# A fused attention and two-MLP kernel: probabilities turned by a transfer in 16-bit halves instead of on the matrix engine, and one relu buffer instead of two

## The reference

```python
# attention: B, H, S, D = 2, 8, 768, 64; block, window = 32, 16
k_sum = k.reshape(B, H, nb, block, D).max(axis=3)
v_sum = v.reshape(B, H, nb, block, D).mean(axis=3)
scores_l = scale * np.matmul(q, k.transpose(0, 1, 3, 2))        # kept where |i - j| < window
scores_s = scale * np.einsum('bhsd,bhnd->bhsn', q, k_sum) + np.log(block)
a = softmax(concatenate([masked scores_l, scores_s], axis=-1))
x = np.matmul(a, concatenate([v, v_sum], axis=2))               # to (1536, 512)
# first MLP, 512 -> 2048 -> 512
h = np.maximum(x @ w_in, 0.0);  y = h * h @ w_out
# second MLP, 512 -> 1024 -> 512
h = y @ w_in2;  solu = h * softmax(h)
out = layer_norm(solu) * g_ln @ w_out2
```

## Time and profile before

| | |
|---|---|
| median of 3 runs | 466.51 us (466.35 to 466.55) |
| profiled execution | 465.99 us, span 464.2 us |
| PE busy | 455.2 us (98%) |
| DVE busy | 261.3 us (56%) |
| ACT busy | 200.9 us (43%) |
| POOL busy | 63.1 us (14%) |
| granted clock | full in all 40 slices |
| attention slots of PE | 46.7 to 236.5 us |
| second MLP | from 323.8 us |

### The profile page before, as it was taken

How to read it: one execution, slowest core, us unless ns; L and a number is a source line. 1 busy time by engine, 2 the same in 40 slices (tenths; PEclk the granted TensorE clock), 3 DMA queues, 4 the chain that set the end, 5 groups by cost and what they waited for, 6 DMA issues and landing times.

```text
span 464.2 us, 6668 instructions
## 1 busy us (share of the span) xinstructions
PE 455.2 (98%) x2526; PEld 375.1 (81%) x2526; DVE 261.3 (56%) x441; ACT 200.9 (43%) x473; POOL 63.1 (14%) x52
## 2 busy tenths in 40 slices
PE   7989999999999999999999999999999999999997
PEld 5778888888888888888888888888888888888875
DVE  4997887866644534434224234444657676767630
ACT  2988555474633433433223233333342345344411
POOL 1420000100000000000000000000135345434510
PEclk9999999999999999999999999999999999999999
DMA  8999487822103511100031111221134334453251
GB/s 284 295 288 256 160 265 227 254 66 59 56 1 111 165 35 26 40 2 1 0 92 45 45 47 49 62 70 46 47 90 58 79 68 69 91 101 82 68 114 45
DMA packets 53120, 45.99 MB, mean 99 GB/s; under 512 B 33376, under 2 KB 38112, under 8 KB 53088
## 3 DMA queue, kind: packets, MB, share of 16 engines
q1 hardware_dynamic: 53088, 45.56, 36.3%
HBM read 33.82 MB, written 5.24 MB: 84 GB/s over the span
## 4 chain that ended last, share of the span: by engine, by line
PE 94%; DVE 2%; DMA 1%; ACT 1%; issue 1%; SPq 0%; POOL 0%; ACTq 0%; DVEq 0%; POOLq 0%
PE bank L993 28%; PE bank L1021 28%; PE bank L1137 14%; PE bank L1119 14%; PE bank L913 4%; PE bank L970 3%; PE bank L938 2%; DMA q_first<-q_head 1%; ACT probs L505 1%; DVE probs L714 1%; DVE probs L696 1%; DVE neg_max L700 1%; PE bank L919 0%; ACT o_sb L661 0%; POOL k_ext L450 0%
## 5 line engine op out<-in xcount | busy, mean ns | idle before, releaser
L727 DVE TENSOR_TENSOR sqr<-relu 128x512 f32<-128x512 f32 x48 | 33.1, 690 | 99.3 <-ACT relu L563 99.3
L563 ACT ACTIVATE relu<-bank 128x512 f32<-128x512 f32 x48 | 28.7, 597 | 119.7 <-PE bank L993 119.7
L993 PE MATMUL bank<-x_hi,win_hi 128*128 128x512 f32 x192 | 76.4, 398 | 0.0
L1021 PE MATMUL bank<-h_hi,wout_hi 128*128 128x512 f32 x192 | 75.1, 391 | 0.0
L993 PE MATMUL bank<-x_hi,win_lo 128*128 128x512 f32 x192 | 74.9, 390 | 0.0
L1021 PE MATMUL bank<-h_hi,wout_lo 128*128 128x512 f32 x192 | 74.7, 389 | 0.0
L993 PE MATMUL bank<-x_lo,win_hi 128*128 128x512 f32 x192 | 74.7, 389 | 0.0
L1021 PE MATMUL bank<-h_lo,wout_hi 128*128 128x512 f32 x192 | 74.7, 389 | 0.0
L489 POOL COPY planes<-cen 128x2048 uint16<-128x2048 uint16 x12 | 33.6, 2798 | 299.8 <-PE bank L1021 244.0
L505 ACT ACTIVATE probs<-probs,neg_max 128x120 f32<-128x120 f32 x96 | 36.6, 382 | 13.5 <-DVE neg_max L700 13.4
L993 PEld LDWEIGHTS bank<-x_hi,win_lo 128*128 128x128 f32 x192 | 36.0, 188 | 7.8
(11 more groups left out here) (79 smaller groups left out, 698.3 us busy)
## 6 DMA issues: line engine op xcount, KB each, us to landing
win_raw<-w_in_t SPq DMA_DIRECT2D x8, 512.0 KB, 6.4
q_sb<-qT SPq DMA_DIRECT2D x16, 256.0 KB, 3.9
wout_raw<-w_out_t SPq DMA_DIRECT2D x8, 512.0 KB, 6.5
win_raw<-w_t SPq DMA_DIRECT2D x8, 512.0 KB, 3.6
v_ext<-vwin SPq DMA_DIRECT2D x16, 192.0 KB, 4.2
out<-o_sb SPq DMA_DIRECT2D x12, 256.0 KB, 2.8
k_ext<-kT SPq DMA_DIRECT2D x12, 192.0 KB, 3.8
k_raw<-kT SPq DMA_DIRECT2D x4, 400.0 KB, 6.0
```

The source lines that it names most:

```text
L563: nc.scalar.activation(relu[:, n % 2, :], up_bank(n), ACT.Relu).then_inc(relu_ok, 1)
L727: nc.vector.tensor_tensor(sqr[:, n % 3, :], relu[:, n % 2, :], relu[:, n % 2, :], ALU.mult)\
L993: last = nc.tensor.matmul(up_bank(n), win[a][:, f * WC + k * P:f * WC + (k + 1) * P], x[b][:, c % 2, k * CH:(k + 1) * CH], start=(k == 0 a ...
L1021: last = nc.tensor.matmul(down_bank(d), wout[a][:, f * WC + d * P:f * WC + (d + 1) * P], h[b][:, n % 3, :], start=(f == 0 and a == 0 and b ...
```

## The change

For units 10 to 23 (BY_DMA = 10, the third unit after the first chunk's eight) the four transposes on PE and the copy on ACT are taken out. In their place:

- GpSimd, `split_probs(u)`: after normalise(u) it copies the 480 float32 columns as low and high 16-bit halves into `halves`, once the transfer of unit u-1 has landed. It stands behind the windows and summaries of the same slot. `halves` has 128 columns a tile, and is cleared once at the start.
- SyncE, `turn_probs(u+2)`: at the end of iteration u, after its loads (and after spread_v at u = 10), it waits for the split and for the join of unit u+1 (for unit 10: for values(9), since `probsT_in` lies in the second half of `probsT`), and issues one transposing transfer of 128 x 1024 16-bit elements.
- DVE, `join_probs(u)`: placed after normalise(u+1) in the slot of unit u-1; it waits for the transfer and for values(u-1), and writes the first half of `probsT`, which all these units use.

Relu has one buffer instead of two: relu(n) on ACT waits for sqr(n-1) and h_hi(n-1). In the second MLP the copy o_sb of token tile 8 is put ahead of the cast lnT_hi of tile 11 instead of behind it; the other tiles keep their order.

```diff
--- before.py
+++ after.py
@@ -71,6 +71,8 @@
     return h + 2 if u % UPC == 0 and u >= 2 * UPC else h
 
 
+
+BY_DMA = UPC + 2
 X_AT = {x_half(u): u for u in range(UPC, UNITS)}
 
 K_AT = {1: 0, 3: 1, 5: 2, 6: 3}
@@ -132,7 +134,7 @@
         parts.close()
         wout_hi = sb(ctx, "wout_hi", [P, F1 * WC], F32R)
         hid = ExitStack()
-        relu = sb(hid, "relu", [P, 2, CH], F32)
+        relu = sb(hid, "relu", [P, CH], F32)
         h_hi = sb(hid, "h_hi", [P, 3, CH], F32R)
 
         squared = ExitStack()
@@ -142,7 +144,7 @@
         hid.close()
 
         o_sb = sb(ctx, "o_sb", [P, 2, DM], F32)
-        sb(ctx, "hid_rest", [P, 8 * CH - 2 * DM], F32)
+        sb(ctx, "hid_rest", [P, 7 * CH - 2 * DM], F32)
         ident = sb(ctx, "ident", [P, P + AVG], F32)
         minus_half = sb(ctx, "minus_half", [P, 1], F32)
         g_sb = sb(ctx, "g_sb", [P, F2], F32)
@@ -154,6 +156,12 @@
         v_ext = sb(att, "v_ext", [P, PPB, TPU * P], F32)
         k_sum = sb(att, "k_sum", [P, PPB, NB], F32)
         probs = sb(att, "probs", [P, 2, UC], F32)
+
+        halves = sb(att, "halves", [P, 2, TPU, P], U16)
+        turned_halves = ExitStack()
+        sb(turned_halves, "probsT_first", [P, TPU * P], F32)
+        probsT_in = sb(turned_halves, "probsT_in", [P, 2, TPU, P], U16)
+        turned_halves.close()
         probsT = sb(att, "probsT", [P, 2, TPU * P], F32)
         neg_max = sb(att, "neg_max", [P, 2, TPU], F32)
         row_sum = sb(att, "row_sum", [P, 2, TPU], F32)
@@ -198,6 +206,7 @@
         vkept_ok = sem("vkept_ok")
         scores_ok, masked_ok, max_ok, exp_ok = sem("scores_ok"), sem("masked_ok"), sem("max_ok"), sem("exp_ok")
         den_ok, rec_ok, norm_ok = sem("den_ok"), sem("rec_ok"), sem("norm_ok")
+        halves_ok, halves_in = sem("halves_ok"), sem("halves_in")
         probsT_ps, probsT_ok, attn_ps = sem("probsT_ps"), sem("probsT_ok"), sem("attn_ps")
         xhi_ok, xlo_ok = sem("xhi_ok"), sem("xlo_ok")
 
@@ -315,6 +324,17 @@
                     sp.dma_start(y_dram[0, c, :, cols], x_hi[:, c % 2, cols].bitcast(F32)).then_inc(y_saved[d], 16)
                     sp.wait_ge(yclo_ok, KD * c + d + 1)
                     sp.dma_start(y_dram[1, c, :, cols], x_lo[:, c % 2, cols].bitcast(F32)).then_inc(y_saved[d], 16)
+
+            def turn_probs(u):
+
+                sp.wait_ge(halves_ok, u - BY_DMA + 1)
+                if u == BY_DMA:
+                    sp.wait_ge(attn_ps, u)
+                else:
+                    sp.wait_ge(probsT_ok, u)
+                sp.dma_start(probsT_in[:, :, :, :].rearrange("p h t q -> p (h t) q"),
+                             halves[:, :, :, :].rearrange("p h t c -> p (h t c)"), transpose=True)\
+                  .then_inc(halves_in, 16)
 
             def load_vw_first(g):
                 h, cols = g // 2, slice((g % 2) * 2 * TPU * P, (g % 2 + 1) * 2 * TPU * P)
@@ -385,6 +405,8 @@
                     spread_v(PPB - 1)
                     load_w(wout_raw, w_out_t, F1 // WG - 1, wout_in)
                     sp.dma_start(g_sb[:, :], g_cols).then_inc(g_in, 16)
+                if u + 2 < UNITS:
+                    turn_probs(u + 2)
 
             def load_w2(g):
                 sp.wait_ge(up_ok, LAST + WG * (g + 1))
@@ -450,9 +472,17 @@
                 nc.gpsimd.tensor_copy(dst, k_sum[:, p, :].unsqueeze(1).to_broadcast([P, TPU, NB]))\
                   .then_inc(kbc_ok, 1)
 
+            def split_probs(u):
+                pool.wait_ge(norm_ok, u + 1)
+                if u > BY_DMA:
+                    pool.wait_ge(halves_in, 16 * (u - BY_DMA))
+                src = probs[:, u % 2, :].bitcast(U16).rearrange("p (t c h) -> p h t c", t=TPU, h=2)
+                nc.gpsimd.tensor_copy(halves[:, :, :, 0:KX], src).then_inc(halves_ok, 1)
+
             nc.gpsimd.memset(idle[:, 0:2 * P], 0.0).then_inc(idle_ok, 1)
             nc.gpsimd.memset(eps_sum[:, :], EPS_SUM).then_inc(eps_ok, 1)
             nc.gpsimd.memset(minus_half[:, :], -0.5).then_inc(half_ok, 1)
+            nc.gpsimd.memset(halves[:, :, :, :], 0)
             windows_k(0)
             summaries_k(0, 0)
             windows_k(1)
@@ -473,12 +503,13 @@
             windows_k(UPC + 2)
             for n in range(LAST):
                 for h in (2 * n, 2 * n + 1):
-                    if h in SLOTS and SLOTS[h][2] is not None and SLOTS[h][2] + 1 < UNITS:
+                    if h in SLOTS and SLOTS[h][2] is not None:
                         u = SLOTS[h][2] + 1
                         if UPB <= u < UPB + PPB:
                             summaries_k(1, u - UPB)
                         if u < UPB:
                             windows_k(u)
+                        split_probs(SLOTS[h][2])
 
             pool.wait_ge(half_ok, 1)
             pool.wait_ge(down_ok, STEPS)
@@ -558,13 +589,14 @@
 
             def hidden(n):
                 act.wait_ge(up_ok, n + 1)
-                if n >= 2:
-                    act.wait_ge(sq_ok, n - 1)
-                nc.scalar.activation(relu[:, n % 2, :], up_bank(n), ACT.Relu).then_inc(relu_ok, 1)
+                if n >= 1:
+                    act.wait_ge(sq_ok, n)
+                    act.wait_ge(hhi_ok, n)
+                nc.scalar.activation(relu[:, :], up_bank(n), ACT.Relu).then_inc(relu_ok, 1)
                 act.wait_ge(relu_ok, n + 1)
                 if n >= 3:
                     act.wait_ge(down_ok, n - 2)
-                nc.scalar.activation(h_hi[:, n % 3, :], relu[:, n % 2, :], ACT.Square).then_inc(hhi_ok, 1)
+                nc.scalar.activation(h_hi[:, n % 3, :], relu[:, :], ACT.Square).then_inc(hhi_ok, 1)
 
             def chunk_y(c):
                 act.wait_ge(down_ok, (c + 1) * F1)
@@ -616,7 +648,7 @@
                 for h in (2 * n, 2 * n + 1):
                     if h % 2 and n + 2 < STEPS:
                         hidden(n + 2)
-                    if h in SLOTS and SLOTS[h][1] is not None:
+                    if h in SLOTS and SLOTS[h][1] is not None and SLOTS[h][1] < BY_DMA:
                         copy_probsT(SLOTS[h][1])
                     if h in X_AT:
                         x_high(X_AT[h])
@@ -632,6 +664,14 @@
             w2_high(F1 - 2)
             w2_high(F1 - 1)
 
+            def scaled(i):
+                act.wait_ge(rstd_ok, i + 1)
+                act.wait_ge(o_ps, i + 1)
+                if i >= 2:
+                    act.wait_ge(o_out[i % 2], 16 * (i // 2))
+                nc.scalar.activation(o_sb[:, i % 2, :], bank[:, 4 + i % 2, :], ACT.Copy, scale=stat[:, i % 8, 8:9])\
+                  .then_inc(o_ok, 1)
+
             for s in range(TT + 4):
                 p, w = s % 2, s % 8
                 if s < TT:
@@ -646,6 +686,8 @@
                     act.wait_ge(cen_ok, s + 1)
                     nc.scalar.activation(solu[:, p, :], cen[:, p, :], ACT.Square, accum_out=stat[:, w, 6:7])\
                       .then_inc(var_ok, 1)
+                if s == TT:
+                    scaled(s - 4)
                 if 1 <= s <= TT:
                     if s == 1:
                         act.wait_ge(down_ok, STEPS)
@@ -653,13 +695,8 @@
                     if s >= 5:
                         act.wait_ge(o_ps, s - 4)
                     nc.scalar.copy(lnT_hi[:, (s - 1) % 4, :], lnT[:, 1 - p, :]).then_inc(lnhi_ok, 1)
-                if s >= 4:
-                    act.wait_ge(rstd_ok, s - 3)
-                    act.wait_ge(o_ps, s - 3)
-                    if s >= 6:
-                        act.wait_ge(o_out[p], 16 * ((s - 4) // 2))
-                    nc.scalar.activation(o_sb[:, p, :], bank[:, 4 + p, :], ACT.Copy,
-                                         scale=stat[:, (s - 4) % 8, 8:9]).then_inc(o_ok, 1)
+                if s >= 4 and s != TT:
+                    scaled(s - 4)
 
         @block.vector
         def _(dve):
@@ -691,8 +728,10 @@
                 if u == 2 * PPB:
                     dve.wait_ge(edge_in, 16)
                 dve.wait_ge(scores_ok, u + 1)
-                if u >= 2:
+                if 2 <= u < BY_DMA + 2:
                     dve.wait_ge(probsT_ps, u - 1)
+                elif u >= BY_DMA + 2:
+                    dve.wait_ge(halves_ok, u - 1 - BY_DMA)
                 nc.vector.scalar_tensor_tensor(probs[:, s, :], scores_bank(u), SCALE,
                                                mask[:, kind * KX:kind * KX + UC], ALU.mult, ALU.add)\
                   .then_inc(masked_ok, 1)
@@ -714,6 +753,12 @@
                 nc.vector.tensor_tensor(v, v, row_rec[:, s, :].unsqueeze(2).to_broadcast([P, TPU, KX]),
                                         ALU.mult).then_inc(norm_ok, 1)
 
+            def join_probs(u):
+                dve.wait_ge(halves_in, 16 * (u - BY_DMA + 1))
+                dve.wait_ge(attn_ps, u)
+                nc.vector.tensor_copy(probsT[0:KX, 0, :].bitcast(U16).rearrange("p (c h) -> p h c", h=2),
+                                      probsT_in[0:KX, :, :, :].rearrange("p h t q -> p h (t q)")).then_inc(probsT_ok, 1)
+
             def x_low(u):
```

(8 more changed lines are left out.)

## The result

The changed kernel takes 463.49 us (median of 4 runs, 462.82 to 464.01) against 466.53 (466.35 to 466.61): ratio 0.9935, 95% interval 0.9919 to 0.9951, so 3.0 us faster. Forecast were 462.9 us, 459.6 to 465.2. The profiled execution has 462.82 us and a span of 460.9, which is 3.3 us less than before.

A forecast was written before the change was run, and what follows sets the result against it. The prediction took the matrix engine, holding 94% of the chain, as the bound. Gains of 6.1 and 0.7 us less stalls of 3.2 us gave -3.6 us: 462.4 profiled, 462.9 us median, range 459.6 to 465.2.

The forecast's parts named there:

- 6.1 us off the matrix engine: Attention slots of units 10 to 23: turning matmuls leave the matrix engine, 13 x 0.44 plus 0.38 us saved.
- 0.7 us at the end: Last output groups: the matrix engine's wait for o_sb of token tile 8 goes, 0.7 us gained.
- Relu, the clearing: 0: Start of the kernel: the single relu buffer and the clearing of halves cost 0 us.
- (1): SyncE's queue: unit 10's transfer, issued behind weights at 58.88, lands at 65.9 us; bounds 65.2 and 69.0.
- (2): Vector engine: join(10) waits from 64.0 till 65.9, ends at 66.6; values(10) wants it at 66.9, no stall.
- (3): Slot of unit 11: join(11) ends at 78.7, values(11) wants it at 76.8, stall 2.0 us; join(10)'s wait passes whole to the chain.
- The meeting of join(10) with split(11): Both released by transfer 10's landing: join(10)'s wait 0.5 to 0.9 us longer, left out of the sum.
- (4): Scores(14): part 3 of v lands at 80.2, sums_k(1,2) ends at 89.8, stall 1.2 us.
- (5): Slots after scores(14): the vector engine waits again, so no further stall of the matrix engine.
- Sum: Whole kernel: gains of 6.8 us less losses of 3.2 us, -3.6 us.
- All hidden: Rival: transfer not held up behind weights and v_next sooner, whole 6.8 us gained, 459.7 us; chance 0.17.
- Slow transfer: Rival: unit 10's transfer lands 9 to 10 us after issue, 465.1 to 466.0 us; chance 0.14.

The follow-up runs named there:

- run with early transfers: Changed kernel with the transfers of units 10 and 11 issued ahead of their iteration's weight tiles, and unit 12's ahead of spread_v: 463.72 us, ratio 0.9936.
- run without joins: Kernel before with one relu buffer, the o_sb copy moved, and splits and transfers of units 10 and 11 that nobody reads: 465.32 us against 466.19, ratio 0.9983.
- run with the late joins doubled: Changed kernel with the join of units 14 to 23 made twice: 464.31 us, ratio 0.9957 to the kernel before.
- run with the end alone: Kernel before with only the copy o_sb of tile 8 put ahead of the cast lnT_hi of tile 11: 465.40 us against 466.59, ratio 0.9969.

## Why the prediction was right, point by point

- **6.1 us off the matrix engine.** Right in kind: L985 has 40 matmuls instead of 96. Of 0.44 us a slot some 0.02 come back, as the groups behind scores now take 2.76 to 2.78 instead of 2.75. From the scores at 110.71 to the 2.94 us group at 234.29 are 123.58 us, which were 127.29 in the chain before (109.24 to 236.53): 3.7 saved where 8 x 0.44 + 0.38 = 3.9 were counted.
- **0.7 us at the end.** The mechanism was right and the term too small: 1.1 us in the chain, 1.2 in the medians. I took the length of the copy for the price of the wait; stopping and starting again cost 0.3 more.
- **Relu, the clearing: 0.** Confirmed for relu by its own run. The clearing of halves takes 0.95 us from 1.05 us on, and ends before the first keys arrive at 3.8.
- **(1) and (2), the landing.** 65.9 was forecast and 66.2 measured, the join at 66.25. One reading was wrong: between 58 and 76 us the vector engine had a third wait, 1.36 us before 62.97 for the exponentials of unit 11. It lies ahead of normalise(11), so nothing was counted from it.

```profile
62.97 0.16 DVE L706 TENSOR_TENSOR row_den<-row_sum,eps_sum 128x4 f32<-128x4 f32 x1 [1.36 <-ACT probs L505]
```

- **(3), values(11).** Join(11) ended at 78.7 as forecast; the wait was 1.6 us and not 2.0, mostly because the matrix engine itself was 0.3 us later from the start of the kernel. That every microsecond of join(10)'s wait goes to the chain was too strong: with the wait of 1.94 gone, values(11) wait 1.1 us less, because part 2 of v then has to be waited for. The meeting of join(10) with split(11), kept for the range, cost the vector engine nothing: join(10) took 0.76 us and the reduction behind it 1.20, as elsewhere.
- **(4), scores(14).** v_next at 80.2 was forecast, and it was 80.25, in part by luck: sums_v(2) ended at 72.9 as counted, but SyncE was busy for 1.47 us with the issue of k_ext and issued v_next at 73.59, 0.8 us late, and it then landed in 6.7 us instead of 7.4. sums_k at 89.8 against 89.8; the wait 0.8 us, plus 0.3 at values(12) just ahead of it, against 1.2.
- **(5), nothing after.** Wrong by 0.2 us: values(13) waited. The term left out is the meeting of GpSimd's split and a vector operation, 0.8 us where they met at 91 us; a second meeting at 99.9 us came behind the join and cost nothing.
- **Sum.** Waits of 2.9 us, and some 0.4 of restarts, against 3.2: -3.3 in the spans, -3.0 in the medians, forecast -3.6. The 0.4 is a remainder: the stretch got 2.5 us shorter, and 6.1 less 0.3 for the longer groups, less 2.9, would be 2.9. The runs of the changed kernel scatter more (462.8 to 464.0). Two of the four show a mean clock of 0.996 (463.39 and 464.01) and two 0.999 (462.82 and 463.59), so part of them probably lose the clock for a moment after a wait, as the run below; no trace of such an execution of this very kernel was taken.
- **What I had not separated.** My prediction named two causes for the two halves of the loss, the landing of transfer 10 and the landing of v_next, and took the second for a consequence of the first. The run with early transfers shows that the second stays when the first is removed, and then the kernel gains nothing: part 3 of v is late because of what stands ahead of it in the queue, not only because it is issued late. The run without joins adds that two transfers more in the queue cost nothing by themselves.
- **The rivals.** All hidden (459.7): not here, but nearly so once the weights stand behind (460.7). Slow transfer: the upper bound of 69.0 for the landing was far off. That TensorE is to be preferred for such a transpose (the Trainium skill, VectorE: DVE Perf Modes, Rules for kernel authors) does not hold for the units from 12 on, where the way by the queue gains a little over 0.4 us of the matrix engine a unit and costs nothing that it waits for. For units 10 and 11, with SyncE's order as it stood, it does: with them included the kernel is 2.8 us slower. With v ahead of the weights they cost nothing any more (460.67), and gain nothing either.

## What to carry to other kernels

Work taken from the busiest engine and given to a transfer is free only where the queue and the engine that receives it have room at that moment, so it pays to switch over from the first unit where they have, and not from the first where it is possible: here 12 units gain nearly twice what 14 do. When a queue is full, changing places among the transfers ahead of a load does not bring that load sooner; look for the next load whose landing somebody waits for, and put behind it those that nobody waits for yet. And in a stretch where an in-order engine has no pause, count a wait in it at full price, from there to the next pause; but when you remove it, look which wait takes its place.

## What the hardware showed that I had not expected

- **GpSimd beside the vector engine.** The split takes 0.99 us once and 1.43 to 1.51 in the next ones; a vector operation with two inputs from SBUF that meets it goes from 0.68 to 1.47 us (91 us), and 0.68 to 1.49 (99.9 us). The Trainium skill (SBUF — State Buffer, SBUF: two separate sides) says that whichever of two such operations starts first keeps the other out for its whole length. The 0.8 us agree better with that than the 0.5 that I took from the earlier trace rows: the square at 91 us ends 0.55 us after the split (90.45 to 91.89), nearly its own 0.68.
- **A stop of the matrix engine costs more than its length.** 0.3 us more at the end of the kernel before, and 0.4 for the four waits of the changed kernel together, if the remainder is all due to it. And in the run with the late joins doubled the matrix engine stood for 1.87 us before 79.49, and then the granted clock fell to the lower of its two levels, 1.2 GHz, for some 3 us. Its windows:

```profile
78.00:79.00 1.00, 0.00 (x0) 0.00 (x0) 0.97 (x3) 1.00 (x3) 0.15 (x1) 1.00 1.18 306
79.00:80.00 1.00, 0.51 (x16) 0.51 (x16) 0.43 (x1) 0.83 (x2) 1.00 (x1) 1.00 1.05 260
80.00:81.00 1.00, 1.00 (x11) 0.93 (x8) 0.29 (x1) 0.37 (x1) 0.28 (x1) 0.68 1.02 346
81.00:82.00 1.00, 1.00 (x6) 1.00 (x6) 0.97 (x2) 0.00 (x0) 0.00 (x0) 0.50 1.03 379
```

  In the profiled execution of the changed kernel a stop of 1.58 us at the same place left the clock at 1.00.
- **The start scatters.** The third up group starts at 41.23 us in the profiled execution before, at 41.51 after, at 41.16 in the run with the end alone and at 42.69 in the run with one relu buffer, whose span of 465.7 us is that scatter and not its edit: the stretch behind it has its length of before.
- **The transfer.** Eight tiles of 128x128 16-bit elements land in 2.7 us where the queue is empty, with 1.23 us of issue; I had 2.2 and 0.95.
